# Attention and two feed-forward stages on one core: TensorE's fillers in the prologue made wide

## The reference

```python
scores = q @ k.T / sqrt(64)            # heads 0-3: the 32 keys up to the query
scores = where(masks, scores, -1e9)    # heads 4-7: every fourth of the last 128
x = softmax(scores) @ v
x_prev = x shifted by one token
xk, xr = mu_k*x + (1-mu_k)*x_prev, mu_r*x + (1-mu_r)*x_prev
x = sigmoid(xr @ w_r) * (max(xk @ w_k, 0)**2 @ w_v)
h = max(x.T @ w_tok1, 0) @ w_tok2;  u = x + h.T
out = u + max(u @ w_ch1, 0) @ w_ch2
```

## Time and profile before

| what | us |
|---|---|
| median of 3 runs | 666.35 |
| the three runs | 663.12, 666.93, 666.35 |
| the profiled execution, its own time | 662.08 |
| span of its trace, first to last instruction | 660.3 |
| TensorE products busy | 651.3 (99%) |
| VectorE, ScalarE, GpSimd busy | 494.1, 320.0, 250.5 |

### The profile page before, as it was taken

The page is one execution under the profiler, slowest core; times in us unless marked ns, Lnnn a source line. Parts: engine busy times, 40 slices in busy tenths (PEclk is TensorE's granted clock), DMA queues, the critical chain, the costliest instruction groups (busy, mean ns, idle before and its releaser), DMA issues.

```text
span 660.3 us, 17201 instructions
## 1 busy us (share of the span) xinstructions
PE 651.3 (99%) x6977; PEld 629.9 (95%) x6977; DVE 494.1 (75%) x825; ACT 320.0 (48%) x677; POOL 250.5 (38%) x313
## 2 busy tenths in 40 slices
PE   7999999999999999999999999999999999999997
PEld 7879999999999999999988999999999999999997
DVE  5679878596676857687793699786887898676764
ACT  3574562635535254535562347564646664433330
POOL 6584664746356474636676440001001121011000
PEclk9999999999999999999999999999999999999999
DMA  9981343232332324078764635758559998979784
GB/s 206 236 202 36 58 83 82 43 66 54 74 82 43 67 55 106 2 141 164 212 144 160 199 144 190 237 188 281 192 189 337 305 352 253 287 220 289 221 218 72
DMA packets 205518, 107.11 MB, mean 162 GB/s; under 512 B 163128, under 2 KB 192960, under 8 KB 205440
## 3 DMA queue, kind: packets, MB, share of 16 engines
q1 hardware_dynamic: 185680, 66.83, 40.0%
q0 software_dynamic: 6224, 33.43, 15.5%
q10 hardware_dynamic: 13536, 5.76, 3.9%
HBM read 67.05 MB, written 38.93 MB: 161 GB/s over the span
## 4 chain that ended last, share of the span: by engine, by line
PE 96%; DMA 2%; DVE 1%; ACT 0%; issue 0%; ACTq 0%; POOL 0%; POOLq 0%; DVEq 0%
PE bank L972 10%; PE bank L974 9%; PE bank L973 9%; PE tq L972 5%; PE tq L974 4%; PE tq L973 4%; PE bank L1579 4%; PE bank L1580 3%; PE bank L1581 3%; PE bank L1810 3%; PE bank L1812 3%; PE bank L1811 3%; PE tq L1579 3%; PE bank L848 3%; PE tq L1580 3%; PE tq L1581 3%
## 5 line engine op out<-in xcount | busy, mean ns | idle before, releaser
L1776 ACT ACTIVATE ck__hi<-ck__raw 128x576 fp32r<-128x576 f32 x84 | 51.5, 676 | 71.3 <-DMA ck__raw<-h_rows 65.6
L1780 DVE TENSOR_TENSOR ck__lo<-ck__raw,ck__hi 128x576 fp32r<-128x576 f32 x84 | 59.8, 749 | 15.8 <-ACT ck__hi L1776 15.5
L1748 POOL DMA_DIRECT2D ck__raw<-h_rows x28 | 14.9, 530 | 149.6 <-PE bank L1581 54.3
L1067 POOL TENSOR_TENSOR k_lo<-kr,k_hi 128x288 fp32r<-128x288 f32 x64 | 56.7, 890 | 24.8 <-ACT k_hi L1063 24.3
L1109 DVE RECIPROCAL rg<-rg 128x288 f32<-128x288 f32 x32 | 61.5, 1923 | 0.0
L1579 PE MATMUL bank<-U__hi,W__hi 128*128 128x288 f32 x192 | 57.1, 297 | 0.1
L1580 PE MATMUL bank<-U__hi,W__lo 128*128 128x288 f32 x192 | 56.6, 295 | 0.0
L1581 PE MATMUL bank<-U__lo,W__hi 128*128 128x288 f32 x192 | 56.4, 294 | 0.0
L972 PE MATMUL bank<-k_hi,WV_hi 128*128 128x288 f32 x184 | 55.4, 301 | 0.0
L973 PE MATMUL bank<-k_hi,WV_lo 128*128 128x288 f32 x184 | 54.3, 295 | 0.0
L974 PE MATMUL bank<-k_lo,WV_hi 128*128 128x288 f32 x184 | 54.1, 294 | 0.0
(11 more groups left out here) (261 smaller groups left out, 2308.6 us busy)
## 6 DMA issues: line engine op xcount, KB each, us to landing
h_rows<-hq SPq DMA_DIRECT2D x24, 1008.0 KB, 5.9
ck__raw<-h_rows POOLq DMA_DIRECT2D x28, 864.0 KB, 5.8
x_turned<-xblocks SPq DMA_DIRECT2D x16, 288.0 KB, 5.2
u_kept<-X SPq DMA_DIRECT2D x4, 1152.0 KB, 5.3
ub<-u_kept POOLq DMA_DIRECT2D x8, 576.0 KB, 7.4
xT_raw<-x_turned SPq DMA_DIRECT2D x4, 1024.0 KB, 5.7
out_x<-ob SPq DMA_DIRECT2D x52, 72.0 KB, 4.9
vt<-in_v SPq DMA_DIRECT2D x70, 48.0 KB, 2.3
```

What stands on the lines that cost most here:

```text
L1067: e.tensor_tensor(lo, t, hi.bitcast(F32), ALU.subtract).then_inc(Z.lo_done, 1)
L1780: e.tensor_tensor(lo, raw, hi.bitcast(F32), ALU.subtract).then_inc(Z.cl_done, 1)
```

## The change

In the prologue, five of the seven groups of fillers change. 7 small ones become 2 small ones and two wide products of 384 columns; 2 become one wide product of 256 columns; three times 3 become one of 384. The group of one and the last group of three stay. A wide product has the identity as its weights and zeros from `mixed` as its moving operand, and writes bank 0 from column 0. It waits for `zeroed` to be at least 1. VectorE gets one memset more, 384 columns of `mixed`, ahead of the others but for `ones`, with an increment of `zeroed`; all other waits on `zeroed` count one more.

```diff
             def scalar(e):
                 if h == 0:
-                    e.wait_ge(Z.zeroed, 3)
+                    e.wait_ge(Z.zeroed, 4)
                 load_head(e, 0, 1, h, v_in[0])
...
                 if n == 0:
-                    e.wait_ge(Z.zeroed, 3)
+                    e.wait_ge(Z.zeroed, 4)
...
                 if n == 0:
-                    e.wait_ge(Z.zeroed, 2)
+                    e.wait_ge(Z.zeroed, 3)
                 e.wait_ge(Z.tq_done, n + 1)
...
+        def keep_warm_wide(n, ps=mlp_ps[0], free=None):
+
+            def tensor(e):
+                e.wait_ge(Z.zeroed, 1)
+                if free:
+                    e.wait_ge(*free)
+                e.matmul(ps[:, 0:n], ident[:, :], mixed[:, P:P + n], start=True, stop=True)
+            return dict(tensor=tensor)
+
...
-                keep_warm(7), transposes(0), evictions(0), load_first_head(0), keep_warm(2), scores(0), mask(0), maximum(0), subtract_max(0),
-                transposes(1), evictions(1), load_first_head(1), keep_warm(3), scores(1), mask(1), maximum(1), subtract_max(1),
-                transposes(2), evictions(2), exponentials(0), keep_warm(3), scores(2), mask(2), sums(0), normalise(0),
+                keep_warm(2), keep_warm_wide(384), keep_warm_wide(384), transposes(0), evictions(0), load_first_head(0), keep_warm_wide(256), scores(0), mask(0), maximum(0), subtract_max(0),
+                transposes(1), evictions(1), load_first_head(1), keep_warm_wide(384), scores(1), mask(1), maximum(1), subtract_max(1),
+                transposes(2), evictions(2), exponentials(0), keep_warm_wide(384), scores(2), mask(2), sums(0), normalise(0),
                 maximum(2), subtract_max(2),
-                transposes(3), evictions(3), exponentials(1), keep_warm(3), scores(3), sums(1), normalise(1), mask(3), maximum(3),
+                transposes(3), evictions(3), exponentials(1), keep_warm_wide(384), scores(3), sums(1), normalise(1), mask(3), maximum(3),
...
-                e.wait_ge(Z.zeroed, 1)
+                e.wait_ge(Z.zeroed, 2)
                 e.activation(stat[0][:, 0:1], stat[0][:, 0:1], ACT.Exp)
...
             e.memset(ones[:, :], 1.0)
+            e.memset(mixed[:, P:4 * P], 0.0).then_inc(Z.zeroed, 1)
             e.memset(stat[0][:, 0:1], 0.0).then_inc(Z.zeroed, 1)
...
-            e.wait_ge(Z.zeroed, 4)
+            e.wait_ge(Z.zeroed, 5)
             main("vector", e)
```

## The result

The changed kernel takes 667.90 us in the median of 22 runs (664.37 to 672.78), the kernel before, run beside it, 663.19 us (22 runs, 661.28 to 667.99). The ratio is 1.0051 with an interval of 1.003 to 1.0072: slower by half a per cent, where I had forecast 0.95 us faster. The profiled execution took 671.63 us, with a span of 669.8.

The account below looks back on a forecast made before the run. TensorE, busy 99% of the span, was taken as the bound. Dearer first fillers +0.40, faster later ones -0.05, the moved hole and what follows -1.30: in all -0.95 us, 666.35 to 665.4 us; range 662.0 to 667.5.

Parts of the forecast that it names:

- The count: TensorE's 1.6 us idle in the fourth score block is a 256-instruction code block's edge, fixed by 437 preceding instructions.
- the hole is not tied to the count: Rival, chance 0.13: the 1.6 us idle stays in the fourth score block; only dearer first fillers count, +0.35 us.
- there and behind it -1.30: Sum's term from the idle gap in the fourth score block onward: weighted values start at 16.8, not 17.73 + 0.35.
- TensorE can go on at 16.3 to 16.65: Code past the moved edge, ahead of the first weighted values, is usable by then, so the gap costs nothing more there.
- its 6.7 us: Time from the previous code edge, 9.22 us, to 15.95, for the next block to be asked for, carried and made usable.
- The code comes later: Rival, chance 0.12: code usable only at 17.7, weighted values start as before, change 0, 666.35 us.
- The clock rises later: Rival, chance 0.07: wide zero products raise TensorE's clock more slowly at the start, some 1.4 us more, 666.8 us.
- A new hole later: Rival, chance 0.08: one of 54 later code edges, all moved by 40 instructions, opens up to 1.6 us; 667.0 us.
- I count no wait: At the first feed-forward product, its last two weight quarters, issued at 19.13, arrive in time; range's end allows 0.5 us.
- the prologue's -0.95: Net gain forecast for the whole change, from weighted values and first feed-forward product starting earlier, in us.

Follow-up runs that it names:

- e1: Changed kernel with 40 instructions given back as waits met long before, at the five places with fewer fillers; ratio 1.0013 to the kernel before.
- e4: The changed kernel once more, unaltered, for a second profile; 664.1 us in its one run.
- e6: Changed kernel with 40 instructions of already met waits between 30 and 45 us, so later edges stand as before; ratio 1.0052 to the kernel before.
- e2: Kernel before with its small fillers and their number, but zeros as moving operand of 16 of the 18; ratio 1.0000.
- e3: Changed kernel with ones in place of zeros in the wide fillers' operand; ratio 1.0069 to the kernel before.
- e9: Changed kernel with five small fillers in the wait ahead of the second weighted values and 20 instructions later on; ratio 1.0000 to the kernel before.
- e5: Kernel before with ten small fillers left out and no wide ones, the same 40 instructions fewer; ratio 1.0055.
- e13: Kernel before with 20 instructions saved ahead of the fourth score block and spent on five fillers in the wait before the second weighted values; ratio 0.9997.
- e10: Kernel before with its last four small fillers moved ahead of the fourth score block, same number of instructions; ratio 1.0018.
- e12: Kernel before with its last three small fillers moved from ahead of the first weighted values into the wait before the second; ratio 1.0003.
- e11: Kernel before with five small fillers added in the wait ahead of the second weighted values; ratio 1.0042.
- e8: Changed kernel with the first two quarters of w_k loaded later, behind values; ratio 1.0052 to the kernel before.

## Why the prediction was wrong

**What held.** The count: the hole is a block's edge, and by 40 instructions fewer it moved in the work and stayed behind instruction 437 of the stream, as e1 and the two counts show. The rival "the hole is not tied to the count" fell. Where the code came early (e4), the stages ran as worked out: transposes at 5.47 (I had 5.4), fourth score block in one piece, first copies into X ending at 18.56 (18.3). VectorE masked at 15.24 in the changed profile, against 16.42, and the first feed-forward product of e6, with neither hole nor fall, started at 23.8 (I had 24.2). The memset cost nothing that shows, zeros against identity made no difference, and a wide product of 384 columns took 0.67 as computed.

**The step that failed** is the sum "there and behind it -1.30", in three terms.

*The latency of the code taken as fixed.* "TensorE can go on at 16.3 to 16.65": it went on at 19.06 in the changed profile and had no hole in e4. I had one profile and made its 6.7 us a constant. Over these profiles the transfer began between 11.0 and 16.2 us. What varied is its start: it began 1.4 to 6.7 us after the edge before it was passed, while from its start to TensorE's going on it was 2.7 to 3.6 us in the ten profiles with a hole. My rival "The code comes later" (0.12) had the right event, but stopped at 17.7 and at a cost of nothing.

*The clock left out.* I had priced half speed only for the start ("The clock rises later", chance 0.07) and not behind the hole. Moving the hole by 40 instructions put the fillers that stood behind it, seven of the eight passes, ahead of it; what follows is the hole, thin products and the 1.2 us for ScalarE's copies. The mean clock is at 0.995 or below in 16 of 22 runs, before in 6 of 29. Its cost is 4.6 - 1.6 = 3.0 us on average, by the measure above, of 4.1 us between the means (667.9 and 663.8). That it comes with the missing 40 instructions and not with the wide zeros alone rests on e1 and e2, with e3 and e6 for the data and the late edges; that work in the wait cures it, on e9. Whether wide products are needed for it beside the moved edge is open: e5 lost only 1.0 us more than before to the clock, apart from its one long run. In the changed profile and in e13 the clock fell within a hole of over 3 us, in e4 behind the wait, without a hole: there are at least these two ways to it, and which the other runs took is not known. That the order of hole and fillers alone decides is only argued: e10 leans that way, e12 shows nothing.

*The late edges.* "A new hole later" had 0.08 in my list and 1.6 us as its price; it is there, 1.3 to 1.65 us in four of five profiles with the late edges moved by 40, and e6 takes it away. I dismissed it by one dense stretch without a hole; that the engine ran ahead there is a property of the place, and I should have gone through all edges moved by 40.

*And the gain is not kept.* In e6, with no hole and no fall, the feed-forward began 1.3 us earlier than before, and the keys of block 4 took 1.7 us back. My sentence "I count no wait" looked at the weights alone, not at the next load of TensorE's stream, and for the weights it was wrong too (1.0 to 1.3 us in e5, e9 and e10, which have the loads as they were). Late hole (0.9) and clock (3.0) make 3.9 of the 4.1 us, each known to about 1 us, so of the prologue's -0.95 nothing is left that can be measured.

*The baseline.* I anchored the level at 666.35, the median of three runs; the same kernel has 663.2 in 22. The profiled execution's 662.08 was the better anchor. With 665.4 as the centre the upper end of 667.5 was too low by 0.4 us; with the right level the miss would have been larger.

The rule of the Trainium skill ("Runtime: NRT & Kernel Launch", section "Instruction fetch mechanics") that fetching of code is hidden is contradicted by e1 and the changed profile together: the hole stands behind the same count of instructions, at two places of the work. The Trainium skill also says ("TensorE: Matmul & The Clock Gate", section "HAM oscillation — how this bites in real kernels") that idle gaps send TensorE back to half clock. The changed profile agrees, with the fall at 18.9 in 3.27 us of standing still; e4, where a wait of 1.2 us was followed by the same, shows that a gap of 3 us is not needed.

## What to carry to other kernels

The number of instructions of a stream is a setting of its own: here removing 40 moved every edge at which code must arrive, and a "free" edit can cost in the place where an edge falls on a dense run of thin products or next to an existing wait. When a kernel keeps TensorE's clock up with fillers, look at what stands between each pair of waits behind the last filler, and try a filler in a wait that is already there (e9 took e6's clock loss away by it, while e11, with the same fillers, had the lowest clock loss and was slower); and take the granted clock of every run, since the mean clock split this 0.6% into its parts when times alone could not. Read the clock loss with and without the longest run: e5's 11.9 us was one run in ten. An early arrival is worth only what the next load of the stream allows.

## What the runs showed of the hardware that was not expected

The transfer that brings TensorE's third block of code began at 11.0 to 16.2 us in the sixteen profiled executions, whose streams before it differ by far less, and twice in one and the same kernel at 12.6 and 11.8 (before), 16.2 and 11.6 (changed). The first stretches at half clock differed as much: 17.1 us in the changed kernel, 13.7 in e3 and e12, 10.2 in e8 and e13, 3.4 in e1, e2 and e4, though TensorE was busy nearly throughout. And the rise at the start came at 5.2 to 8.1 us after equal or nearly equal work; at 5.2 (changed profile) it hid the dearer first fillers: the transposes began at 5.36 with fast passes, and the fourth score block at 13.70, against 13.72 before.
